# A first load of 128 rows, issued as one transfer or as two of 64 rows

## The reference, cut to what matters

```python
# q, k, v: (8, 8, 576, 64) f32; g_norm: (64); phi: (512, 32); w1: (8, 512, 1024); w2: (8, 1024, 512)
kv = np.einsum('bhsd,bhse->bhde', k, v)
out = np.einsum('bhsd,bhde->bhse', q, kv)
rms = np.sqrt(np.mean(out * out, axis=-1, keepdims=True) + 1e-06)
x = (out / rms * g_norm).transpose(0, 2, 1, 3).reshape(4608, 512)

logits = x @ phi
d = softmax over the 4608 tokens of logits          # one column per slot
slot_input = (d.T @ x).reshape(8, 4, 512)
slot_out[e] = np.maximum(slot_input[e] @ w1[e], 0) @ w2[e]
c = softmax over the 32 slots of logits             # one row per token
result = c @ slot_out                               # (4608, 512)
```

## Time and profile before

| | us |
|---|---|
| median of 3 runs | 171.91 |
| lowest, highest | 171.82, 171.95 |
| the profiled execution | 171.88 |
| its span, from first to last instruction | 170.6 |

### The profile page before, as it was taken

One profiled execution on the slowest core, in us unless ns is written; L12 is line 12 of the kernel. 1 busy time (PEld: TensorE's weight loads), 2 busy tenths in 40 slices (PEclk: granted clock), 3 DMA queues, 4 the chain that ended last, 5 costly groups with the idle time before them and its releaser, 6 DMA issues.

```text
span 170.6 us, 4246 instructions
## 1 busy us (share of the span) xinstructions
PE 150.1 (88%) x1838; PEld 105.1 (62%) x1838; DVE 86.8 (51%) x185; ACT 89.0 (52%) x230; POOL 59.6 (35%) x73
## 2 busy tenths in 40 slices
PE   7887897989999899999899998989999989999500
PEld 3466776979678888896697674345566533455200
DVE  1122156283677266762946698823888136306600
ACT  3127576796975887859759864202223034406600
POOL 7000708648357745377382679400000004000000
PEclk9999999999999999999999999999999999999985
DMA  5999999999999999999999999999999999999997
GB/s 181 422 432 419 444 414 441 474 416 444 458 427 408 445 441 415 434 392 459 423 442 407 444 403 417 440 446 407 430 426 446 440 442 392 421 419 429 419 421 323
DMA packets 4365, 71.65 MB, mean 420 GB/s; under 512 B 790, under 2 KB 790, under 8 KB 922
## 3 DMA queue, kind: packets, MB, share of 16 engines
q1 hardware_dynamic: 3994, 71.18, 97.8%
q0 software_dynamic: 352, 0.20, 0.4%
HBM read 61.94 MB, written 9.44 MB: 418 GB/s over the span
## 4 chain that ended last, share of the span: by engine, by line
PE 50%; DMA 24%; ACT 12%; DVE 6%; SPq 2%; issue 1%
PE psum L214 50%; DMA arena<-in_kv_dram 13%; DMA arena<-in_w_dram 10%; ACT bd L214 3%; ACT sq L214 3%; ACT xall L214 2%; SPq L214 2%; DVE logits L214 1%; DVE ms L214 1%; ACT part L214 1%; ACT arena L214 1%; ACT d L214 1%; DVE part L214 1%; ACT r L214 1%; DVE acc L214 1%
## 5 line engine op out<-in xcount | busy, mean ns | idle before, releaser
L214 PE MATMUL psum<-bd,arena 128*128 128x192 f32 (+1 forms) x320 | 56.1, 335 | 1.9 <-ACT bd L214 1.5
L214 PEld LDWEIGHTS psum<-bd,arena 128*128 128x128 f32 (+1 forms) x320 | 45.4, 179 | 8.6 <-ACT bd L214 2.8
L214 DVE TENSOR_REDUCE ms<-sq 128x16 f32<-128x1024 f32 (+1 forms) x19 | 22.1, 1162 | 32.7 <-ACT sq L214 32.5
L214 POOL TENSOR_TENSOR part<-part,r 128x512 f32<-128x512 f32 x17 | 17.8, 1048 | 49.5 <-DVE r L214 49.5
L214 POOL TENSOR_TENSOR xall<-xall,r 128x512 f32<-128x512 f32 x34 | 34.7, 1042 | 0.0
L214 ACT ACTIVATE sq<-psum 128x512 f32<-128x512 f32 x36 | 21.5, 598 | 12.8 <-PE psum L214 12.7
L214 PE MATMUL psum<-arena 128*64 128x64 f32 (+1 forms) x640 | 21.7, 226 | 3.2 <-DMA arena<-in_kv_dram 2.6
L214 PEld LDWEIGHTS psum<-arena 128*64 128x64 f32 (+1 forms) x640 | 19.0, 137 | 8.6 <-DMA arena<-in_kv_dram 3.8
L214 ACT COPY xall<-psum 128x512 f32<-128x512 f32 x34 | 20.7, 608 | 0.0
L214 ACT COPY part<-psum 128x256 f32<-128x256 f32 (+1 forms) x38 | 13.7, 359 | 11.8 <-DVE part L214 10.6
L214 DVE TENSOR_REDUCE logits<-part 128x64 f32<-128x512 f32 (+1 forms) x18 | 17.8, 989 | 0.0
(11 more groups left out here) (80 smaller groups left out, 126.4 us busy)
## 6 DMA issues: line engine op xcount, KB each, us to landing
arena<-in_w_dram SPq DMA_DIRECT2D x4, 4096.0 KB, 23.6
arena<-in_w_dram SPq DMA_DIRECT2D x4, 2048.0 KB, 20.3
arena<-in_t_dram SPq DMA_DIRECT2D x1, 6912.0 KB, 36.1
arena<-in_w_dram SPq DMA_DIRECT2D x2, 3072.0 KB, 22.7
arena<-in_kv_dram SPq DMA_DIRECT2D x2, 2304.0 KB, 23.6
arena<-in_kv_dram SPq DMA_DIRECT2D x1, 4608.0 KB, 43.0
arena<-in_kv_dram SPq DMA_DIRECT2D x1, 3584.0 KB, 32.6
arena<-in_kv_dram SPq DMA_DIRECT2D x3, 1152.0 KB, 13.5
```

The costliest lines, as they stand in the source:

```text
L214: inst = getattr(engine, method)(*args, **kwargs)
```

## The change

The first transfer is cut between rows 63 and 64. SyncE issues rows 0 to 63, at the place where it issued the whole; ScalarE issues rows 64 to 127, and this stands in the code ahead of its table load. The other seven transfers of the start are as they were, on SyncE.

```diff
-    nc.sync.dma_start(arena[:, : HEAD + 2304], first_in)
+    nc.sync.dma_start(arena[:64, : HEAD + 2304], first_in[:64])
+    nc.scalar.dma_start(arena[64:, : HEAD + 2304], first_in[64:])
     load_row(KV_AT[0] + 9, kv_in[0, :, 2304:])
```

## The result

| | before | changed |
|---|---|---|
| median, us (4 runs each) | 171.93 | 174.53 |
| lowest, highest | 171.82, 172.08 | 174.39, 174.94 |
| the profiled execution | 171.88 | 174.49 |
| its span | 170.6 | 173.2 |

The ratio is 1.0154, with a 95% interval of 1.0136 to 1.0173. The forecast was no change (171.9, range 171.4 to 173.8); the time lies 0.7 us above the range, in the region of the rival "half of the rows is a slow target".

What follows compares the result with a forecast made beforehand. The prediction took one unbroken stream of transferred bytes to bound the kernel. From the profiled 171.88 us, 0.03 under the median of 171.91, its terms 0 + 0 + 0 + 0 + 0 left 171.9 us, range 171.4 to 173.8.

Steps and rivals of the forecast that it cites:

- no change: Whole kernel: the time stays within 171.55 to 172.25 us, an idle or queued second half included; chance 0.42.
- half of the rows is a slow target: First load into `arena`: engines writing the same closed half get in each other's way; 1.5 us more, 173.4 us; chance 0.36.
- What bounds the kernel: From about 2.9 us to the last store: one stream of bytes without a hole; shifting it x moves the end about x.
- The prediction's own sign: Wait at 26.78 us: if its start moves by x and the end does not, the stream is not the bound.
- The cover: First 26 us: engine delays that leave the stream unmoved are repaid at 26.78 us, if under some 1.3 us.
- The issues: Start: ScalarE's added issue takes 0.4 us, SyncE's of 64 rows 0.3 to 0.4 instead of 0.39; cost at the end 0.
- The table load's cover: ScalarE's start: 5.64 us idle before its first work covers a table load ending near 2.4 instead of 2.01 us.
- The waits: TensorE's first product and VectorE's second gphi operation: one more wait, well under 0.1 us; cost at the end 0.
- The first bytes: Ramp before 2.90 us: the only possible gain, from nothing up to 0.9 us; taken as 0.
- The shape: First load as two 64-row transfers: cost 0, taken from 64-row stores near the end draining at 425 GB/s.
- The rival's price: First load at half rate: 3.0 us more if halves go strictly in turn, halved to 1.5 us for two queues.

## Why the prediction was wrong

**What bounds the kernel: right.** The end follows the stream of bytes. Adding 2.76 us to the stream behind an undisturbed start cost 2.8 us; keeping TensorE's clock up won nothing; and a late start of TensorE alone cost 0.8 us at the median, 1.9 in the execution whose trace is shown. The prediction's own sign came as well: the products that began at 26.78 us began at 29.69, 2.9 us later, and the end moved by 2.6.

**The cover: right in kind, too small for this.** Some 1.3 us of lateness would be repaid at 26.78 us, it said. TensorE came 3.5 us late and ran its first work at half clock, which no step had reckoned with. By itself that cost the 0.8 to 1.9 us of the whole load issued by ScalarE; in the changed kernel the stream was as late, and it cost nothing on top (with the clock kept up the time was the same).

**The issues: 0.4 us each was too low.** They took 0.56 and 0.60 us. I had expected the issue of half the rows to be as long or shorter; it is longer, from SyncE as from ScalarE (two in 1.24 us from SyncE alone). The table load's cover (5.64 us) held without trouble. The waits cost nothing either: VectorE's two operations on gphi take 0.58 us with the second wait between them, as without it.

**The first bytes: wrong, and bounded on one side only.** The value was 0, with gains of up to 0.9 us above it and "nothing" as the lower bound. Spread over all rows, where the region plays no part, the kernel was slower by 0.3 us with two issuers and by 0.8 with one, and the first packet came 0.3 us later: a loss, which the bound had excluded. The reason given for 0 (both leave the barrier at 0.73 us) spoke against a gain, and said nothing of a loss.

**The shape: this is the step that failed.** It took 0 from the nearest row, the stores of 64 rows at 425 GB/s, and had itself said what separates them from the change: they take every second row and they read. The first difference is enough: loads of even and odd rows run at 394 GB/s, closed halves at 231. In the property that counted, the stores were like a load of all 128 rows. (The second was not tried: no run stores a closed half. And the earlier trace rows hold more than these stores, since from about 153 us on a store of all 128 rows drains; from 147 to 153 us alone the rate is 420 GB/s, so the reading of a full rate stands.) So the row was no evidence against the rival, though the prediction counted it as such: the rival got 0.36 behind the 0.42 of no change, and the term was put at 0.

**The rival's price: 1.5 us, measured 2.6.** Its mechanism was right, and its signs came as listed (first products at 7.5 us or later, a rate of 300 or less). Its price halved the 3.0 us, on the thought that with two queues the engines would work on both halves at once. They hardly did: ScalarE's half landed 3.3 us before SyncE's, its packets had all started by 4.80 us and SyncE's began at 4.25, and one issuer with the halves in a row gave the same time (174.57). The full price of 3.0 us is nearer to what it cost, and the range, cut off inside this rival at 173.8, missed for that reason. By the Trainium skill's page "SBUF — State Buffer" ("Can I just issue two DMAs to hit both halves?") the load was estimated at 6.0 us and the kernel at 174.9: the changed kernel agrees within 0.4 us, and its first load runs from the first packet's start at 2.06 us to the last one's end at 8.48, 6.4 us. Why the two queues took turns by whole halves here, while a whole load by ScalarE shared the engines with SyncE's loads from the start, stays open (even and odd rows with two issuers came in two blocks as well); a run that makes two halves alternate was not tried.

## What to carry to other kernels

Best here was not to cut the first load at all. If a transfer has to be cut, every piece should reach rows of both halves (0 to 63 and 64 to 127): every second row cost this kernel 0.3 to 0.8 us, and two closed halves 2.6, nearly the 3.0 of one more whole load. A cut by columns was not run. When the nearest row of a trace stands in for a case that it doesn't show, ask which property of it the price hangs on, and price the case by the difference if that property differs. And read the rate beside the busy share: from 2.90 to 6.20 us both kernels show engines that are busy all of the time, and only the GB/s tell that one of them moves about half as much.

## What the runs showed of the hardware

- Loads into rows of one half run at 208 to 266 GB/s by stretch, with 64 or with 32 rows; 64 rows over the border between 63 and 64, or every second row, at 322 to 394 at the start; whole loads at 403 to 428. The transfer engines are about as busy in all of them (shares of 0.89 to 1.13).
- As the first issue of an engine, a load of 64 rows takes 0.56 to 0.60 us and one of 128 rows of about the same length 0.38 to 0.40. The first packet behind it starts at 2.06 to 2.18 us, against 1.75 or 1.76.
- TensorE's granted clock went from 2.4 to 1.2 GHz at about 8.5 us, after it had idled from 5.98, and was back at 2.4 by 15.5 us, after work from 9.65 on.
